# Moving three of six low-part subtractions of the output weights to other places in their engines' orders

## What is computed

```
scores = q @ k.T / sqrt(64) + bias(relu(x @ w1 + b1) @ w2)     # 4 x 8 heads, 576 x 576, head size 64
attn   = softmax(scores) @ v                                   # -> x: 2304 tokens x 512
gate   = sigmoid(x @ w_gate);  val = x @ w_val                 # 512 -> 1536
out    = (gate * val) @ w_out                                  # 1536 -> 512, float32
```

## Time and profile before

| | |
|---|---|
| runs | 737.61, 737.66, 739.21 us (median 737.66) |
| the profiled execution's own time | 737.71 us |
| its span, first to last instruction | 735.9 us |
| mean granted TensorE clock | 1.000 |
| busy share of the span | TensorE 97%, VectorE 69%, ScalarE 63%, GpSimd 48% |
| line 1055 (VectorE's low parts of output weights) | 4 instructions, 680 to 1782 ns |
| line 670 (GpSimd's) | 2 instructions, 1358 and 1751 ns |

### The profile page before, as it was taken

How to read it: one execution, slowest core, us unless ns; L and a number is a source line. 1 busy time by engine, 2 the same in 40 slices (tenths; PEclk the granted TensorE clock), 3 DMA queues, 4 the chain that set the end, 5 groups by cost and what they waited for, 6 DMA issues and landing times.

```text
span 735.9 us, 14243 instructions
## 1 busy us (share of the span) xinstructions
PE 714.7 (97%) x4962; PEld 588.1 (80%) x4962; DVE 507.7 (69%) x1065; ACT 463.9 (63%) x934; POOL 354.1 (48%) x473
## 2 busy tenths in 40 slices
PE   7779999999999999999999999999999999999998
PEld 4337777677777666789889998998899899989997
DVE  7996777777777888738814868784178758705841
ACT  7998777777778777767516752763367437516720
POOL 0004555554569898755564625562155355504500
PEclk9999999999999999999999999999999999999999
DMA  6886232222362222133310241211022422201002
GB/s 178 217 207 149 65 104 75 68 67 76 98 230 75 67 67 69 42 102 127 118 42 30 86 143 72 73 58 58 1 78 67 158 73 68 76 0 58 30 10 76
DMA packets 56886, 63.64 MB, mean 86 GB/s; under 512 B 22128, under 2 KB 48240, under 8 KB 56816
## 3 DMA queue, kind: packets, MB, share of 16 engines
q1 hardware_dynamic: 56384, 62.65, 28.6%
q10 hardware_dynamic: 432, 0.09, 0.1%
HBM read 42.67 MB, written 9.44 MB: 71 GB/s over the span
## 4 chain that ended last, share of the span: by engine, by line
PE 82%; DVE 11%; issue 3%; ACT 2%; DMA 1%; POOL 0%; ACTq 0%; DVEq 0%; POOLq 0%
PE f_ps L1372 20%; PE z_ps L1303 19%; PE v_ps L1265 10%; PE y_ps L1303 10%; DVE feats L936 7%; PE so_ps L1211 7%; PE x_ps L1303 5%; PE ty_ps L1222 4%; PE tx_ps L1232 3%; PE so_ps L1206 2%; PE tx_ps L1245 1%; ACT probs L754 1%; DVE sum_eps L976 1%; DVE neg_scores L961 1%; PE tx_ps L1235 1%
## 5 line engine op out<-in xcount | busy, mean ns | idle before, releaser
L1303 PE MATMUL z_ps<-xc,wc 128*128 128x384 f32 x864 | 165.5, 336 | 0.6 <-DVE wc L1018 0.5
L1303 PEld LDWEIGHTS z_ps<-xc,wc 128*128 128x128 f32 x864 | 150.5, 188 | 4.0 <-ACT keep L781 1.6
L754 ACT ACTIVATE probs<-neg_scores,neg_max 128x576 f32<-128x576 f32 x144 | 110.8, 770 | 46.0 <-DVE neg_max L961 45.6
L586 POOL TENSOR_SCALAR probs<-probs,recip 128x512 f32<-128x512 f32 x144 | 99.0, 699 | 79.5 <-DVE recip L981 79.5
L961 DVE CUSTOM_DVE_ANT_0 neg_scores<-so_ps,bias 128x576 f32<-128x576 f32 x128 | 92.2, 755 | 5.3 <-PE so_ps L1194 3.9
L613 POOL TENSOR_TENSOR wc<-t_raw,wc 128x512 fp32r<-128x512 f32 x37 | 48.8, 1318 | 87.6 <-ACT wc L773 87.6
L1303 PE MATMUL y_ps<-xc,wc 128*128 128x384 f32 x432 | 86.6, 334 | 0.5 <-DVE sig L1034 0.5
L781 ACT ACTIVATE keep<-z_ps 128x384 f32<-128x384 f32 x108 | 52.9, 490 | 52.3 <-PE z_ps L1303 51.7
L1372 PE MATMUL f_ps<-wo_h,h_h 128*128 128x512 f32 x210 | 82.1, 391 | 0.7 <-issue 0.7
L599 POOL TENSOR_TENSOR t_raw<-w_stage 128x512 f32<-128x512 f32 x36 | 50.4, 1399 | 66.2 <-DVE wc L1018 66.2
L1372 PE MATMUL f_ps<-wo_h,h_l 128*128 128x512 f32 x210 | 82.0, 391 | 0.0
(11 more groups left out here) (125 smaller groups left out, 1427.0 us busy)
## 6 DMA issues: line engine op xcount, KB each, us to landing
qk_whole<-in_qk SPq DMA_DIRECT2D x16, 608.0 KB, 4.7
w_stage<-in_w_gate SPq DMA_DIRECT2D x18, 512.0 KB, 3.5
w_stage<-in_w_val SPq DMA_DIRECT2D x18, 512.0 KB, 3.6
bias<-bias_rows SPq DMA_DIRECT2D x12, 576.0 KB, 5.1
out<-out_sb SPq DMA_DIRECT2D x17, 256.0 KB, 2.0
v_main<-in_v SPq DMA_DIRECT2D x32, 128.0 KB, 2.3
x_whole<-attn_transposed SPq DMA_DIRECT2D x9, 384.0 KB, 6.0
wo_whole<-in_w_out SPq DMA_DIRECT2D x6, 512.0 KB, 4.6
```

The source lines that it names most:

```text
L586: nc.gpsimd.tensor_scalar(row, row, recip[:, stat(s, place)], 1.0, ALU.mult, ALU.mult).then_inc(normed, 1)
L754: nc.scalar.activation(probs[s % RING][:, place, :], neg_scores[:, shift_place(s, place), :], ACT.Exp, bias=neg_max[:, stat(s, place)], sc ...
L1303: last = nc.tensor.matmul(quad_ps[bank][n % 2][:, 0:CH], wc[:, n % 2, wl, W_PARTS.index(wp), t, :], xc[:, X_PARTS.index(x), xl, t, :], sta ...
```

## The change

The six subtractions of 128x512 that make the low parts of tiles 0 to 5 stay what they are and on the engines that they are on; three of them change their place. VectorE's second one of quad 3 (tile 1) and its second one of quad 5 (tile 3) move from behind `sum_block(n - 1, "12")` to behind `low_w(n + 1, "B22")`. GpSimd's low part of tile 4 moves from pass 5 to pass 6, where it stands directly ahead of that of tile 5. No DMA, no semaphore and no count is changed.

```
@@ -301,7 +301,7 @@
         WO_HIGH = {2: (0, 1), 3: (2, 3), 4: (4, 5)}
         WO_LOW = {3: (0, 1), 5: (2, 3)}
-        WO_LAST = {5: (4,), 6: (5,)}
+        WO_LAST = {6: (4, 5)}
@@ -1110,7 +1110,7 @@
                     sum_block(n - 1, "12")
-                for f in WO_LOW.get(n, ()):
+                for f in WO_LOW.get(n, ())[:1]:
                     low_wo(f)
@@ -1125,6 +1125,8 @@
                 if n < QUADS - 1:
                     low_w(n + 1, "B22")
+                for f in WO_LOW.get(n, ())[1:]:
+                    low_wo(f)
                 if n % PHQ == PHQ - 1:
```

## The result

The changed kernel takes 741.52 us (median of 6 runs, 739.43 to 742.08) against 737.82 us before, slower by 0.5% by these medians. The ratio that takes in all runs, which is close to that of their means, is 1.0041 with a 95% interval of 1.0028 to 1.0054: slower by 0.4%. (The ratios of the experiments are of this kind too.) The median is 2.3 us more than the 739.2 that was forecast, beyond the 0.3% within which I had put a chance of 0.69, and within 0.02 of 741.5, the upper end of the range. Its profiled execution alone took 739.43 us, which is the forecast almost to the tenth. The six runs explain the rest by themselves: the one of 739.43 us has a mean granted TensorE clock of 1.000, the other five, 740.65 to 742.08 us, have 0.998 or 0.995.

The account below looks back on a forecast made before the run. TensorE was taken to bound the kernel, so only the first output piece's start counted. Upstream gains spent ahead of one longer wait left it 1.44 us later: 737.71 + 1.44 = 739.2 us, range 736.9 to 741.5.

Parts of the forecast that it names:

- What bounds the kernel: TensorE, busy 97%; the change is worth only what it does to the first output piece's start, 363.69 us.
- The price of a held instruction: VectorE and GpSimd take whole-instruction turns on two SBUF inputs; VectorE's subtraction takes 1.32 to 1.78 us instead of 0.68.
- Quad 3: Tile 1 to the quad's end: P1(4) starts some 0.6 us earlier; gain alone 0 to 0.6.
- Pass 5 without tile 4: GpSimd's line 599 ends 1.69 us earlier, P3(4)'s 0.67 gap goes, line 613 starts at 358.34; alone gains about 1.
- Quad 5: Moved tile 3 ends at 365.02, so the output piece starts at 365.13, 1.44 us later; alone costs about 2.
- list of turns: From VectorE's tile 2 to B1(6), VectorE and GpSimd alternate; the chain to tile 3 holds three GpSimd turns, not two.
- The sum: Whole kernel: 737.71 us plus 1.44 for the later output piece gives 739.2 us, +0.2%.
- rival 2: TensorE's clock falls in the 3.4 us gap before the output piece: +4.2, 742.0 us; chance 0.10.
- 1: Upstream gain does not arrive: line 613 stays at 360.03, quad 5 is 1.69 later, +3.1, 740.8 us; chance 0.13.
- 3: GpSimd's two low parts lie outside VectorE's quad-5 stretch: piece at 362.9, -0.8, 736.9 us; chance 0.17 shared with 4.
- 4: Tile 3 does not release the output piece, so only upstream gain shows, 0.95 at most: 736.8; chance 0.17 shared with 3.

Follow-up runs that it names:

- GpSimd behind tile 3 and quad 5 undone: Changed kernel with tile 3 back in its old place and GpSimd waiting for VectorE's tile 3 before tiles 4 and 5; ratio to before 0.9979.
- GpSimd behind B22: Changed kernel with tile 3 back in its old place and GpSimd waiting for VectorE's B22 of quad 6 before tiles 4 and 5; ratio to before 0.9960.
- quad 5 alone: Kernel before with only tile 3 moved to the end of its quad; ratio to before 1.0055.
- both low parts at the end: Changed kernel with VectorE's tile 2 also moved to the end of quad 5, ahead of tile 3; ratio to before 1.0043.
- the filled gap: Changed kernel with 12 unused matmuls on TensorE ahead of the first output piece; median 739.22 us, ratio to before 1.0026.
- quad 3 alone: Kernel before with only tile 1 moved to the end of its quad; ratio to before 0.9987.
- GpSimd behind tile 3: Changed kernel with GpSimd waiting for VectorE's tile 3 before its low parts of tiles 4 and 5; ratio to before 0.9998.

## Why the prediction was right or wrong, point by point

- *What bounds the kernel.* Right. A change of the piece's start came out in the time: +1.97 gave +1.9 us, -1.02 gave -1.1, -1.49 gave -1.4. The one exception in the runs is the kernel with GpSimd behind tile 3 and quad 5 undone, where a new wait arose behind the piece. With GpSimd behind B22 the piece starts equally early and the whole gain arrives (-2.28, -2.4 us). So "behind the first output piece there is nothing that could take a delay back or pass on a gain" holds for the change itself, but not where GpSimd's turns hold what stands behind the piece.
- *The price of a held instruction.* Right in both directions. After the change GpSimd's pair at line 670 took 3.27 us, and the three held instructions of VectorE 1.32, 1.65 and 1.75; with GpSimd out of the way two of them went back to 0.55 and 0.68. That is what the Trainium skill, page "SBUF — State Buffer", section "SBUF: two separate sides", says of the exclusive lock.
- *Quad 3.* -0.60 forecast; P1(4) no longer waits, the moved low part starts at 346.81 and the next sum at 348.52 (346.76 and 348.46 were written). Alone it carries 0.50 to the piece.
- *Pass 5 without tile 4.* Right: line 613 at 358.52 (358.34 forecast), no wait of P3(4), "about 1" of gain alone against 1.02. In the changed kernel P2(5) was 0.42 ahead (0.4 taken).
- *Quad 5.* "Costs about 2" alone: 1.97. With the other moves it costs 3.05, which the prediction's list of turns covers. Together 365.13 was forecast for the piece and 365.31 came. Line 613's start, 0.18 late, is enough for that.
- *The sum.* It comes out as 739.15 when it is redone, and it was right for an execution whose clock stays up: +1.44 against +1.62 at the piece, 739.2 against 739.43 us.
- *The step that failed* is the chance of rival 2, 0.10. I had written "no row here shows a fall" and counted that as evidence that there would be none; but the trace had no standstill of that length behind steady work, so it could not speak either way. The fall came in five of the six runs. Its price was sized right for the dearest falls (2.8 forecast, 2.4 + 0.3 measured at quad 5 alone; 742.0 us forecast, 742.04 and 742.06 in the two runs at clock 0.995). The runs at 0.998 are cheaper: 740.65 and 741.01 us, 1.2 and 1.6 above the run that kept its clock, and the one fall at 0.998 that a trace shows, with both low parts at the end, cost 1.4. With the falls the result lies beyond 0.3%, on the side to which I gave 0.28. The range was drawn to end below rival 2. That the median came out at its end and not well outside is luck: it lies halfway between a run at 0.998 (741.01) and one at 0.995 (742.04). The runs agree with the warning of the Trainium skill, page "TensorE: Matmul & The Clock Gate", section "Why this matters for your kernels", against idle gaps between bursts of matmuls, which deserved more weight than the silence of the trace. They go beyond it: the clock fell at waits of 2.3 and 2.7 us too, shorter than the gaps that the page warns of.
- *Rivals 1, 3 and 4.* 1: line 613 did come early, so it does not apply. 3: did not happen by itself, but forcing it gave -0.58. 4: excluded by the filled gap, where the view names line 1055.

What stays open: why a run starts up in one group or the other, why the clock falls in some runs of the same kernel and not in others, the gain of 0.7 us in the times of quad 3 alone where its trace shows 0.50, and what a wait between 1.5 and 2.3 us would do.

## What to carry to other kernels

Work that is moved to the end of a stage is not hidden by the fact that its engine has idle time: ask which wait counts it, and what stands ahead of it now, held instructions at their held length. Where two engines take turns, list the turns between the two ends of the chain, and put those that nobody waits for behind the last instruction that is waited for, far enough that they don't hold the next one. And behind a standstill of TensorE of 2.3 us or more the clock fell in 17 of 21 runs here, which costs on top of its length, so price it with a fall of the clock included, unless runs show that it stays up.

## What was not expected of the hardware

- The granted clock fell behind waits of 2.3 us and 2.7 us in four of five and four of six runs. A fall cost 2.7 us in the trace with a wait of 2.7 us, as much as the wait itself, and 1.4 us in the one with a wait of 3.7 us and both low parts at the end.
- The first instructions of the program did not take the same time in every execution, whatever the kernel. The twelve warm-up matmuls of 128x192 took 3.84 us in the profiled execution before and 4.21 us in that of GpSimd behind tile 3, and ScalarE's first `qk_h` copy began at 17.51 and 18.88 us. The clock view reads 1.00 in both.
